# A repeated instruction order of one whole chunk instead of a quarter of it, with two semaphores split, in a convolution and two gated layers on one core

## What is computed

```
x1  = causal depthwise convolution of x, 7 taps, per head softmax(weight)      # 8192 tokens x 192
g   = sigmoid(x1 @ w_gate) * (x1 @ w_val)                                      # 1536 columns
x2  = g @ w_out
h   = x2 @ w_in                                                                # 2048 columns
f   = (a0 + a1 h + a2 h^2 + a3 h^3) / (1 + |b0||h| + |b1| h^2 + 1e-6)
out = f @ w_out2                                                               # 8192 x 192
```

## Time and profile before

| | |
|---|---|
| median of 3 runs | 1367.0 us (1366.86 to 1368.48) |
| profiled execution, its own time | 1366.47 us |
| its span, first to last instruction | 1364.7 us |
| busy: PE, DVE, ACT, POOL | 1285.5 (94%), 1245.7 (91%), 1122.5 (82%), 637.5 us (47%) |
| granted TensorE clock, mean | 0.988 |

### The profile page before, as it was taken

How to read it: one execution, slowest core, us unless ns; L and a number is a source line. 1 busy time by engine, 2 the same in 40 slices (tenths; PEclk the granted TensorE clock), 3 DMA queues, 4 the chain that set the end, 5 groups by cost and what they waited for, 6 DMA issues and landing times.

```text
span 1364.7 us, 16882 instructions
## 1 busy us (share of the span) xinstructions
PE 1285.5 (94%) x5440; PEld 1026.4 (75%) x5440; DVE 1245.7 (91%) x1201; ACT 1122.5 (82%) x1278; POOL 637.5 (47%) x337
## 2 busy tenths in 40 slices
PE   4889999999999999999999999999999999999876
PEld 3767787777778777777777778777777877778654
DVE  7759999999999999999999999999999999998998
ACT  5468889888888888889888888888888888888774
POOL 1423545454454553554554454554454455455532
PEclk9989999999999999999999999999999999999978
DMA  7100000010100001000010100001010000000000
GB/s 202 38 0 20 1 12 21 1 31 0 31 0 11 20 0 31 0 19 12 4 27 0 31 0 12 19 0 31 0 31 0 8 23 0 19 0 12 1 12 12
DMA packets 15960, 23.66 MB, mean 17 GB/s; under 512 B 2240, under 2 KB 10048, under 8 KB 15936
## 3 DMA queue, kind: packets, MB, share of 16 engines
q1 hardware_dynamic: 14160, 21.30, 5.6%
q10 hardware_dynamic: 1776, 2.06, 0.6%
HBM read 13.13 MB, written 6.29 MB: 14 GB/s over the span
## 4 chain that ended last, share of the span: by engine, by line
PE 55%; DVE 22%; issue 9%; POOL 8%; ACT 5%; DVEq 0%; DMA 0%; POOLq 0%; SPq 0%; ACTq 0%
POOL frac_low L733 8%; PE up_ps L306 7%; PE up_ps L307 6%; PE up_ps L308 6%; PE up_ps L310 6%; PE up_ps L309 6%; DVE denom L903 5%; PE acc_main L313 5%; DVE denom L893 5%; PE acc_main L314 4%; PE acc_tail L317 4%; PE acc_tail L315 4%; PE acc_main L316 4%; DVE frac_high L884 2%; DVE numer L874 2%
## 5 line engine op out<-in xcount | busy, mean ns | idle before, releaser
L733 POOL TENSOR_TENSOR frac_low<-denom,seed 128x1024 fp32r<-128x1024 f32 x126 | 334.3, 2653 | 626.4 <-DVE denom L903 591.8
L724 POOL TENSOR_TENSOR gated_low<-gated,gated_high 128x512 fp32r<-128x512 f32 x192 | 286.5, 1516 | 67.4 <-ACT gated_high L545 67.4
L306 PE MATMUL up_ps<-x_high,up_high 128*128 128x512 f32 x640 | 255.5, 399 | 43.5 <-DVE x_low L935 15.9
L307 PE MATMUL up_ps<-x_high,up_low 128*128 128x512 f32 x640 | 252.3, 394 | 0.0
L308 PE MATMUL up_ps<-x_low,up_high 128*128 128x512 f32 x640 | 252.3, 394 | 0.0
L310 PE MATMUL up_ps<-x_tail_low,up_tail 128*128 128x512 f32 x640 | 251.5, 393 | 0.0
L309 PE MATMUL up_ps<-x_tail_high,up_tail 128*128 128x512 f32 x640 | 251.3, 393 | 0.0
L556 ACT ACTIVATE seed<-up_ps,coef 128x1024 f32<-128x1024 f32 x128 | 143.0, 1117 | 85.5 <-POOL frac_low L733 46.8
L866 DVE TENSOR_TENSOR numer<-up_ps,numer 128x1024 f32<-128x1024 f32 x128 | 156.3, 1221 | 52.9 <-ACT numer L565 32.3
L306 PEld LDWEIGHTS up_ps<-x_high,up_high 128*128 128x128 f32 x640 | 121.3, 189 | 81.3 <-DVE denom L856 17.4
L565 ACT ACTIVATE numer<-up_ps,coef 128x1024 f32<-128x1024 f32 x128 | 153.9, 1202 | 25.0 <-DVE denom L903 18.4
(11 more groups left out here) (88 smaller groups left out, 2273.7 us busy)
## 6 DMA issues: line engine op xcount, KB each, us to landing
x_raw<-x_chunks SPq DMA_DIRECT2D x16, 393.0 KB, 3.1
out_chunks<-out_main SPq DMA_DIRECT2D x16, 256.0 KB, 2.1
tail_twice<-conv SPq DMA_DIRECT2D x60, 64.0 KB, 2.0
out_chunks<-tail_part SPq DMA_DIRECT2D x16, 128.0 KB, 2.3
...
```

The lines of the kernel that those rows point to most:

```text
L306: nc.tensor.matmul(acc, up_high[:, cols], x["high"][:], start=True, stop=False)
L307: nc.tensor.matmul(acc, up_low[:, cols], x["high"][:], start=False, stop=False)
L724: nc.gpsimd.tensor_tensor(gated_low[:, b], gated[:, b], gated_high[:, b], ALU.subtract).then_inc(gated_low_done, 1)
L733: nc.gpsimd.tensor_tensor(ring(frac_low, j, 2, LOW_RING), ring(denom, j), ring(seed, j), ALU.mult).then_inc(frac_low_done, 1)
```

## The change

The instructions are the same, and so is what they compute. Three things differ.

1. **Order.** `period` with its four like windows is replaced on each engine by `chunk(i)`, a list of one whole chunk, written out call by call, in which every window has an order of its own. The head (chunks 0 and 1) is written out as well; chunk 2 is laid out flat, 3 to 14 run in the loop, 15 is flat. In the head the order of TensorE, ScalarE and GpSimd is that of before; on VectorE some taps stand elsewhere. The drain is that of before, but for a few calls that the list of the last chunk now holds, or no longer holds.
2. **Where the list is cut.** The body of the loop now starts in the middle of window 3: TensorE's begins with `up_gate(i - 1, 3, 2)`, VectorE's with `gate(i - 1, 3, 2)`.
3. **Semaphores.** `x1_low`, which counted both low parts of x1, becomes `x1_main_low` and `x1_tail_low`. `out_copied` becomes `out_main_copied` and `out_tail_copied`. The first `down_gated` of a chunk now waits for `x1_main_low` and `x1_tail_summed` in place of both low parts.

```diff
-        x1_low = sem("x1_low")
+        x1_main_low, x1_tail_low = sem("x1_main_low"), sem("x1_tail_low")
...
-        def periods(eng, period):
-            for i in range(3):
-                period(i)
-            with eng.Fori(3, chunks - 1) as i:
-                period(i)
-            period(chunks - 1)
+        def chunk_loop(eng, chunk):
+            chunk(FIRST_LOOPED)
+            with eng.Fori(FIRST_LOOPED + 1, chunks - 1) as i:
+                chunk(i)
+            chunk(chunks - 1)
...
-                        pe.wait_ge(x1_low, 2 * i)
+                        pe.wait_ge(x1_main_low, i)
+                        pe.wait_ge(x1_tail_low, i)
...
                     if k == 0:
-                        after(pe, x1_low, 2 * i)
+                        after(pe, x1_main_low, i)
+                        after(pe, x1_tail_summed, 2 * i)
...
+            def chunk(i):
+                gate(i - 1, 3, 2)
+                high_fraction(i - 1, 3, 0)
+                split_x0_tail(i)
+                quadratic(i, 0, 0)
...
+                rest(i - 1, 3, 0)
+                conv_tap(i + 1, 0)
+                split_x1_tail(i)
+                split_x1_main(i)
...
```

More of the change, by code:

```diff
@@ L25 @@
 H_BEHIND = 5
+FIRST_LOOPED = 2
 RING = 4
@@ L752, in _ @@
+            chunk_loop(pool, chunk)
+            split_gated(chunks - 1, 2, 1)
+            split_gated(chunks - 1, 2, 2)
             low_fraction(*late(-6))
@@ new lines, in _ @@
+            conv_tap(2, 3)
+            gate(1, 1, 0)
+            gate(1, 1, 1)
+            gate(1, 1, 2)
+            quadratic(1, 2, 0)
+            cubic(1, 2, 0)
+            quadratic(1, 2, 1)
+            denominator(1, 2, 0)
+            cubic(1, 2, 1)
+            high_fraction(1, 1, 0)
+            denominator(1, 2, 1)
+            product(1, 1, 0)
+            high_fraction(1, 1, 1)
+            rest(1, 1, 0)
+            conv_tap(2, 4)
+            gate(1, 2, 0)
+            gate(1, 2, 1)
@@ new lines, in _ @@
+            gate(1, 2, 2)
+            product(1, 1, 1)
+            conv_tap(2, 5)
+            rest(1, 1, 1)
+            quadratic(1, 3, 0)
+            cubic(1, 3, 0)
+            conv_tap(2, 6)
+            quadratic(1, 3, 1)
+            denominator(1, 3, 0)
+            cubic(1, 3, 1)
+            high_fraction(1, 2, 0)
+            denominator(1, 3, 1)
+            product(1, 2, 0)
+            high_fraction(1, 2, 1)
+            rest(1, 2, 0)
+            gate(1, 3, 0)
+            gate(1, 3, 1)
```

777 lines of the change are left out of this document (557 added, 220 removed).

## The result

| | before | after |
|---|---|---|
| median | 1366.9 us | 1398.5 us (1393.6 to 1400.8, 4 runs) |
| ratio to before, 95% interval | | 1.0224 (1.0192 to 1.0256) |
| profiled execution, its own time | 1366.47 us | 1396.45 us |
| its span | 1364.7 us | 1394.6 us |

The changed kernel is 2.2% slower. The direction was forecast; 1380 us was not enough, and the range, up to 1392, did not hold it.

The account below looks back on a forecast made before the run. TensorE was taken to set the time (floor 78.5 us a chunk), VectorE close behind; stalls of 3.6 make 82.1 against 81.2, 11.7 us over 13 chunks plus 1 for the last: 1380 us, range 1350 to 1392.

Parts of the forecast that it names:

- the exclusion: A VectorE operation with two SBUF inputs and a GpSimd one keep each other out and take turns.
- its three places: x1's splits, window 1 and the body's beginning, where GpSimd's frac_low holds VectorE up for 1.5, 2.2 and 2.2 us.
- the entry: Head and first chunk of the new body: head put at 0, with 2 us either way; chunks at 0.9 us more each.
- slower matmuls behind the 2.0 us stall: TensorE behind its wait for x1's split: 0.1 us added, making the stall 2.1 us a chunk.
- stalls of 2.1, 0.7, 0.4 and 0.4 us: TensorE's waits at up_h(i,1,0), up_gate(i,1,0), up_h(i,2,0)'s second tile and up_gate(i,2,0): 3.6 us a chunk.
- B and C gone, A stays: Rival: VectorE's back-to-back operations keep GpSimd out; 80.7 us a chunk, 1360 us; chance 0.2 for B or C missing.
- B: Window 1: GpSimd waits for high_fraction, then has its turn, and tap 2 loses 2.2 us on VectorE.
- C: Body's beginning: the second frac_low holds split_x0_tail from 7.2 to 9.4 us, so the first quadratic stands at 10.0.
- A: x1's splits: GpSimd starts beside tap 0, so split_x1_tail waits; cost 1.5 us on VectorE.
- C's 0.6 us on the path: First quadratic of a chunk at 10.0 where its operands would allow 9.4; of 2.2 us 0.6 stay on the path.
- One more of either each chunk: Rival: split_gated under high_fraction (up to 1.1 us) or A at 2.2; 82.7 to 83.2 a chunk, 1388 to 1394; chance 0.2.
- The drain and the last chunk: Drain unchanged: 0, with 2 us either way; last chunk has no taps, so 1 us (0 to 2).

Follow-up runs that it names:

- e6: On e3's kernel, tap 2 multiplies x without adding the taps before it (one SBUF input in place of two): 1352.8 us, ratio 0.9897.
- e1: On the changed kernel, tap 0 moved back behind gate(i,0,2), so split_x1_tail follows rest(i-1,3,0) at once: 1372.9 us, ratio 1.0048.
- e3: On the changed kernel, the edits of e1 and e2 together: 1364.2 us, ratio 0.9981.
- e2: On the changed kernel, split_x0_tail(i) moved from ahead of quadratic(i,0,0) to behind cubic(i,0,0): 1388.2 us, ratio 1.0155.
- e4: On the changed kernel, 7 extra matmuls without use fill TensorE's stall before the low parts of x1: 1394.4 us, ratio 1.0196.
- e5: On the changed kernel, the edits of e2 and e4 together: 1386.4 us, ratio 1.0142.
- e12: On e4's kernel, product(i-1,3,0) moved from ahead of cubic(i,0,0) to behind it: 1401.3 us, ratio 1.0251.
- e8: On e3's kernel, VectorE's head order: denominator(1,3,1) ahead of high_fraction(1,2,0), product(1,2,1) and rest(1,2,1) ahead of gate(1,3,0): 1366.8 us, ratio 0.9998.
- e13: e3's kernel with taps 2 and 1 moved too (1349.87 us); first looped chunk: gates before product(1,2,1) and rest(1,2,1), quadratic before high_fraction: 1349.7 us.
- e14: On e13's kernel, TensorE's down_gated(1,2,1) also moved ahead of up_gate(1,3,2): 1350.2 us, ratio 0.9873.

## Why the prediction was right and where it was wrong

What bounds the kernel, the exclusion and its three places were right. Three terms of the sum failed: the entry into the new body was put at 0.9 us like any other chunk and took 4.8; slower matmuls behind the 2.0 us stall were put at 0.1 us a chunk and took 1.5 us more in each of four chunks, 6 us in all; and a collision of `product(i-1,3,0)` with `split_gated` was put at nothing and took 1.17 us in four of twelve chunks, 4.7 us.

- **The exclusion, right.** All three places were found where the layout put them, with the durations that it gave: 2.26, 3.15 and 2.88 us against 2.2, 3.2 and 2.9. Tap 0 took its 1.00 to 1.01 us beside GpSimd too (14 of the 15 had GpSimd beside them; tap 2 in e6 as well). The Trainium skill ("SBUF — State Buffer", section Who interferes with whom), which the prediction weighed, lets `tensor_scalar` take the shared ports when its operands meet certain conditions; the trace settles it for this form alone, which was not slowed.
- **The steady chunk, right in sum.** The forecast was 82.1 and stalls of 2.1, 0.7, 0.4 and 0.4 us; undisturbed chunks take 82.34, and by TensorE's starts (a wait with the slower matmuls behind it) the stalls are 2.0 on x1, 0.7 at `up_gate(i,1,0)`, 0.4 at the second tile of `up_h(i,2,0)`, 0.5 at `up_gate(i,2,0)` and some 0.3 of small ones. That the forecast of 80.7 for "B and C gone, A stays" is also e1's and e3's chunk is chance: they have A gone, and B stays.
- **C's 0.6 us on the path, wrong term.** It is 0.1. I took 9.4 as the time at which `quadratic`'s operands would be there; e2 shows VectorE waiting 2.02 of the 2.2 us anyway. A is worth more by as much: 1.6 to 1.7 us net (after to e1).
- **"One more of either each chunk", the rival that came nearest.** It had a chance of 0.2, for `split_gated` under `high_fraction`. The collision came with the product behind it, at 1.2 us, and not each chunk but in 4 of 12. That rival's 1388 to 1394 us also came nearest to the time, partly by luck: it knew neither the clock nor the entry. The layout had VectorE's rows and GpSimd's `frac_low`, but not its `split_gated`, so it couldn't show the pair; and with errors of some tenths it could not have decided a race of 0.03 us. Such a pair belongs in the range at its full price.
- **The clock, missing.** The sum gave the 2.0 us stall only 0.1 us for slower matmuls, as behind before's stalls of up to 1.3 us, which no fall followed. Here a fall followed in 4 of 13 chunks, at 1.5 us each, 6 us in all. e4, e5 and e12, which fill the stall, have none.
- **The entry, mis-sized.** The new body was taken to cost the first chunk 0.9 us like every other; it cost 4.8. The old order of the head and the new one of the body meet at a seam that I had not laid out: there VectorE had no gap from 124 to 149 us, with 1.2 and 1.75 us of exclusion in the product at 134.33 and the `high_fraction` at 138.62. Which of these the 4.8 us come from stays open: e8, e13 and e14 each took one of TensorE's waits away and won nothing clear of the noise.
- **The drain and the last chunk, right:** behind matmul 4680 (12 x 340 + 600) 1.5 us are added, where 1 us was forecast for the last chunk and nothing for the drain.

Added up for the profiled executions, forecast at 1379.2 and measured at 1396.45, the forecast lacks 3.9 at the entry, 4.7 by the race, 6 by the clock, 12 x 0.19 = 2.3 in the chunks as such (1.09 us over before in place of 0.9) and 0.5 at the end: 17.4 for the 17.25 us. The median lies 2.1 us above its profiled execution in place of 0.8, which is the rest of the 18.5.
